# Attention and mixture of experts on one core: the attention loop re-ordered into two-step periods

## What is computed

```python
# q, k, v: (2, 8, 768, 64), proj: (64, 6)
q_bucket = sum(((q @ proj) > 0) * 2 ** arange(6));  k_bucket likewise
scores = q @ k.T / 8, set to -1e9 where q_bucket != k_bucket
attn = softmax(scores);  x = attn @ v            # 16 heads in all
x = moe(x, w_gate, w_noise, noise, w1, w2)       # 8 experts, the top 2 of each token
out = gelu_like(x @ w_in) @ w_out
```

## Time and profile before

| what | us |
|---|---|
| median of 3 executions (lowest, highest) | 1029.27 (1027.99, 1030.33) |
| profiled execution, its time / its span | 1037.7 / 1035.6 |
| TensorE matmul busy | 920.9 (89%) |
| VectorE / ScalarE / GpSimd busy | 428.7 / 348.8 / 416.7 |
| first transposes of step 0 / of step 12 / last normalise ends | 27.6 / 65.9 / about 304 |
| share of TensorE in the chain that ended last | 73% |

### The profile page before, as it was taken

How to read it: one execution, slowest core, us unless ns; L and a number is a source line. 1 busy time by engine, 2 the same in 40 slices (tenths; PEclk the granted TensorE clock), 3 DMA queues, 4 the chain that set the end, 5 groups by cost and what they waited for, 6 DMA issues and landing times.

```text
span 1035.6 us, 15081 instructions
## 1 busy us (share of the span) xinstructions
PE 920.9 (89%) x4789; PEld 746.9 (72%) x4790; DVE 428.7 (41%) x756; ACT 348.8 (34%) x616; POOL 416.7 (40%) x247
## 2 busy tenths in 40 slices
PE   3699999999975389969999999999389999999998
PEld 3566666666643368858888888888279999999996
DVE  4567776677535812212222222222354333333222
ACT  1576677666734011111111111111223232323222
POOL 1222110000028585799594857689695001000000
PEclk8899999999998589989999999999789999999999
DMA  7444653356014279744352525245432011000000
GB/s 161 114 123 110 159 137 85 94 138 168 1 76 162 81 254 343 242 151 155 112 165 94 162 81 172 89 154 162 134 130 82 21 51 38 33 0 0 31 1 31
DMA packets 73237, 116.45 MB, mean 112 GB/s; under 512 B 31920, under 2 KB 33968, under 8 KB 73200
## 3 DMA queue, kind: packets, MB, share of 16 engines
q1 hardware_dynamic: 60592, 86.61, 28.0%
q0 software_dynamic: 4400, 14.42, 4.8%
q10 hardware_dynamic: 8208, 14.95, 4.4%
HBM read 73.49 MB, written 23.59 MB: 94 GB/s over the span
## 4 chain that ended last, share of the span: by engine, by line
PE 73%; DVE 7%; POOL 7%; DMA 6%; SPq 2%; issue 2%; ACT 2%; POOLq 0%; ACTq 0%; DVEq 0%
PE psS L726 13%; PE psT L683 12%; PE psS L667 11%; PE psS L741 9%; PE psV L565 6%; PE psT L554 4%; PE psV L741 4%; PE psS L543 4%; POOL W L433 3%; POOL W L431 2%; DMA x_sb<-x_dram,gather_i 2%; DVE W L796 2%; PE psS L692 2%; PE psM L530 2%; DMA staged<-in_moe_w 2%
## 5 line engine op out<-in xcount | busy, mean ns | idle before, releaser
L431 POOL TENSOR_TENSOR W<-staged,ones_col 128x1024 fp32r<-128x1024 f32 x80 | 152.7, 1909 | 167.9 <-DMA staged<-in_moe_w 103.8
L433 POOL TENSOR_TENSOR W<-staged,W 128x1024 fp32r<-128x1024 f32 x80 | 192.8, 2410 | 6.3
L667 PE MATMUL psS<-W,xT_hi 128*128 x448 | 144.4, 403 | 2.0 <-DVE xT_lo L969 2.0
L726 PE MATMUL psS<-x2T_hi,W 128*128 (+1 forms) x512 | 134.0, 343 | 1.6 <-DVE x2T_lo L987 1.6
L683 PE MATMUL psT<-W,hT_hi 128*128 x448 | 124.5, 410 | 9.2 <-POOL W L433 9.2
L802 DVE TENSOR_REDUCE neg_max<-psS 128x1 f32<-128x768 f32 x96 | 91.6, 954 | 48.9 <-PE psS L543 48.0
L1038 ACT ACTIVATE prob<-psS,exp_arg 128x768 f32<-128x768 f32 x96 | 95.5, 994 | 32.8 <-DVE exp_arg L805 32.7
L543 PE MATMUL psS<-W 128*128 128x384 f32 x384 | 93.4, 366 | 10.7 <-DMA W<-k_hi 9.3
L726 PEld LDWEIGHTS psS<-x2T_hi,W 128*128 128x128 f32 x512 | 94.5, 191 | 6.8 <-issue 2.0
L683 PEld LDWEIGHTS psT<-W,hT_hi 128*128 128x128 f32 x448 | 81.2, 191 | 24.7 <-issue 9.4
L1047 ACT ACTIVATE probT<-psT 128x768 f32<-128x768 f32 x96 | 78.1, 813 | 61.0 <-PE psT L554 59.5
(11 more groups left out here) (170 smaller groups left out, 1295.2 us busy)
## 6 DMA issues: line engine op xcount, KB each, us to landing
staged<-in_moe_w SPq DMA_DIRECT2D x64, 512.0 KB, 3.5
xs_dram<-x_sb SPq DMA_DIRECT2D x31, 256.0 KB, 4.8
x_in<-xs_dram ACTq DMA_DIRECT2D x29, 256.0 KB, 2.7
ys_dram<-y_sb ACTq DMA_DIRECT2D x28, 256.0 KB, 2.4
W<-q_hi SPq DMA_DIRECT2D x32, 192.0 KB, 3.4
W<-k_hi SPq DMA_DIRECT2D x32, 192.0 KB, 3.7
staged<-in_moe_w_in SPq DMA_DIRECT2D x8, 512.0 KB, 3.6
staged<-in_moe_w_out SPq DMA_DIRECT2D x8, 512.0 KB, 3.4
```

The lines of the kernel that those rows point to most:

```text
L431: nc.gpsimd.tensor_tensor(W[:, at:at + CH], staged[:, n % 2], ones_col[:].to_broadcast([P, CH]), ALU.mult).then_inc(s_whi, 1)
L433: nc.gpsimd.tensor_tensor(W[:, at + BLOCK:at + BLOCK + CH], staged[:, n % 2], W[:, at:at + CH].bitcast(F32), ALU.subtract).then_inc(s_spli ...
L667: mm = nc.tensor.matmul(psS[:, 0, half], x[:, c * P:(c + 1) * P], W[:, bass.ds(slot + (w + c * F + half * 512), 512)], start=c == 0 and n ...
L726: mm = nc.tensor.matmul(psS[:, 0, f % 2, 0:GN], W[:, at:at + P], x[:, bass.ds(buf + c * GN, GN)], start=c == 0 and n == 0, stop=c == DC - ...
```

## The change

TensorE's and VectorE's orders are rewritten in periods of two steps, n even. On TensorE a period is: transposes of n, a unit, at a head's start `back`, `weighted`, transposes of n+1, scores of n+3, a unit, scores of n+4. On VectorE it is: statistics of n+2, `collect`, the unit of step n-1, `normalise`, the unit of step n, statistics of n+3. ScalarE keeps its order apart from where the units' copies fall. Units 0 to 3 of a pair move to the last four steps of the pair two before it, units 4 to 7 to steps 0, 2, 3 and 5 of the pair before it (the table `AHEAD`), and units 0 to 3 of pair 1 stand ahead of step 0's transposes. No instruction is added or removed, and the programs of SyncE and GpSimd are as before.

```diff
+        AHEAD = (-4, -3, -2, -1, 0, 2, 3, 5)
         def unit_at(n):
-            return n // PS + 1, n % PS
+            for pr in (n // PS + 1, n // PS + 2):
+                if pr < PAIRS and n - PS * (pr - 1) in AHEAD:
+                    return pr, AHEAD.index(n - PS * (pr - 1))
+            return None
...
         # tensor
             for n in range(2):
                 scores(n)
-            for n in range(STEPS):
+            for n in range(-4, 0):
+                unit(*unit_at(n))
+            transposes(0)
+            scores(2)
+            for n in range(0, STEPS, 2):
                 hd, t = divmod(n, NT)
-                if n + 2 < STEPS:
-                    scores(n + 2)
-                transposes(n)
-                pr, u = unit_at(n)
-                if pr < PAIRS and u < UNITS:
-                    unit(pr, u)
+                if n:
+                    transposes(n)
+                if unit_at(n):
+                    unit(*unit_at(n))
                 if t == 0 and hd >= 2:
                     back(hd - 2)
-                if t % 2 and hd:
+                if hd:
                     weighted(hd - 1, t // 2)
+                transposes(n + 1)
+                if n + 3 < STEPS:
+                    scores(n + 3)
+                if unit_at(n + 1):
+                    unit(*unit_at(n + 1))
+                if n + 4 < STEPS:
+                    scores(n + 4)
...
         # vector
-            for n in range(STEPS):
+            for n in range(-4, -1):
+                unit(*unit_at(n))
+            for n in range(0, STEPS, 2):
                 hd, t = divmod(n, NT)
+                if n + 2 < STEPS:
+                    statistics(n + 2)
                 if t == 0 and hd >= 2:
                     collect(hd - 2)
-                if t == 1 and hd >= 2:
+                if unit_at(n - 1):
+                    unit(*unit_at(n - 1))
+                if t == 0 and hd >= 2:
                     normalise(hd - 2)
-                if n:
-                    pr, u = unit_at(n - 1)
-                    if pr < PAIRS and u < UNITS:
-                        unit(pr, u)
-                if n + 2 < STEPS:
-                    statistics(n + 2)
+                if unit_at(n):
+                    unit(*unit_at(n))
                 if t == 2 and hd:
                     denominators(hd - 1)
+                if n + 3 < STEPS:
+                    statistics(n + 3)
```

More of the change, by code:

```diff
@@ L1056, in _ @@
                 evac(n)
-                pr, u = unit_at(n)
-                if pr < PAIRS and u < 4:
-                    unit(pr, u)
+                if unit_at(n) and unit_at(n)[1] < 4:
+                    unit(*unit_at(n))
             attention_over(act)
```

## The result

The changed kernel takes 1074.12 us (median of 4 executions, 1065.88 to 1078.97), the kernel before 1029.8 in the same comparison: a ratio of 1.042, 95% interval 1.034 to 1.049. The forecast was 1073 in 1060 to 1090. The total came out within 1.2 us, but not by the forecast's own sum: it left out a term of 13.9 us, and terms that it had too high made up for it. The four executions of the changed kernel lie 13 us apart, and those of before 6.

The account below looks back on a forecast made before the run. TensorE was taken to set the attention's pace, with new waits behind VectorE's strict order. Front 12.8, pairs 1 and 2 12.0, pairs 3 to 5 12.0, pair 6 2.0, pair 7 4.6: 43.4 on 1029.3 gives 1073, range 1060 to 1090.

Parts of the forecast that it names:

- Offset 0: Periods are named by their first step's offset in the pair; this one, the pair's start: 8.1 to 8.2 us, 5.42 before.
- offset 4: Period without a head's start or units 0 to 3: falls from 5.80 to 4.85 us, one lump fitting in its slack.
- The circle: At offset 4, scores, reduction, exponential, evacuation, transposes and next scores form a 4.83 us latency that takes back the 0.57 gain.
- +4.0: Added us per pair, 37.9 against 33.9, from the six periods' waits; counted for pairs 1 to 5.
- rival 2: TensorE's clock falls at 14 heads' starts, some 1.5 us each, +21 in all: 1094 us; chance 0.12.
- late q: Scaled q reaches unit 0, now four steps earlier, 2.7 us late; 2.0 counted in pairs 1 and 2, 2.5 at the front.
- Front: Four units ahead of step 0 put T(0) at 42.1 and step 12 at 78.7 against 65.9: +12.8 us.
- The end: Last pairs of the attention: pair 6, without units 0 to 3, +2.0 us; pair 7, with two heads' starts, +4.6.
- Faster: Rival 3: VectorE's statistics are over before T(n), so waits at offsets 0, 6 and 10 go: about 1025 us; chance 0.03.
- little change: Rival 4: half the heads' waits overlap the 4.83 latency, leaving part of the front's cost: 1029 to 1045 us; chance 0.05.
- q in time: The forecast's waits without lateness of the scaled q: 1066 us; chance 0.14.
- rival 1: The chunk lands sooner or GpSimd is ahead, so scaled q is not late: 1066 us; chance 0.14.

Follow-up runs that it names:

- the fillers: The changed kernel with useless transposes of the identity put on TensorE in the waits at each head's start: 1065.34 us, ratio 1.034 to the kernel before.
- Turning GpSimd's order: GpSimd scales the next pair's q ahead of splitting the weight chunk: 1064.84 us in the changed kernel, 1025.3 in the kernel before.
- the split of `weighted`: The kernel before with `weighted` cut into six pieces, one a step, and the last two units a step later: 1019.83 us, ratio 0.989.

## Why the prediction was right, and where not

- **Right, and shown: what sets the time.** The heads' starts. Undone alone they give back 32 us of the 44.5, their falls of the clock with them. VectorE kept its written order in the rows shown, so `collect` did wait behind the statistics.
- **Right in size: each period's waits**, where the clock held. Offset 0 8.2 forecast, 7.8 measured; 2: 5.43, 5.35; 4: 4.85, 4.83; 6: 7.7, 7.5; 8: 5.1, 5.04; 10: 6.65, 6.33. At offset 4 the number was right, and the reason was not: 4.83 is TensorE's own work with a lump in it, 90.27 to 95.10 in the timeline without a wait. The circle from scores over exponential and evacuation to transposes, forecast at 4.83, shows in the plain periods of pair 7, and is 4.70:

```profile
304.19 0.82 PE L559 MATMUL psT<-ident,prob 128*128 128x128 f32 x6
...
306.80 0.85 PE L559 MATMUL psT<-ident,prob 128*128 128x128 f32 x6 [0.34 <-ACT probT L1065]
...
308.89 0.82 PE L559 MATMUL psT<-ident,prob 128*128 128x128 f32 x6
```

  The second transposes wait 0.34 for the evacuation, the first no longer. A plain period is thus 0.15 shorter than before, not the same. Each of offsets 0, 6 and 10 was forecast 0.2 to 0.4 high: statistics hold VectorE for 1.07 (154.44 to 155.51) where 1.18 was counted, and a copy for 0.47 (to 155.98) where it was 0.56. So without falls a pair is +3.0 (7.8 + 5.35 + 4.83 + 7.5 + 5.03 + 6.33 = 36.8), not the **+4.0** of the sum.
- **Wrong: the clock, a term that the sum does not have.** It stood as rival 2, with 0.12 and 14 falls at 1.5. The profiled execution shows 9 falls of 1.3 to 1.7, 13.9 us, and the fillers take them away with the waits left in place. The row on which I had set it aside, 298 to 304 with 1.00, had 1.36 us idle in 6.0 in short pieces; the heads' starts idle for 2.3 in 7.8 (rival 2 had said 3 in 8.2).
- **Wrong: late q in pairs 1 and 2, 2.0 each.** Nothing in pair 1, 0.2 in pair 2. The chain took 10.8 us instead of 13.5, as the chunk landed sooner, and the slower head ahead of it left more time. The mechanism is real: it appears with 2.87 as soon as the heads' wait is gone, and with 10.8 and 13.0 us periods when the table stands alone. In pair 0 it was +1.95 (6.99 for 5.04), where I had 2.5.
- **Front +12.8: measured +11.2**, T(0) at 41.98 for 42.1. That start was right by luck: the first unit came at 35.0 where 36.1 was counted, and the units were 2.0 to 2.2 us apart where 1.85 was. And the four units ahead of T(0) are only half of the reason: without them step 12 is 4 us later still. What binds the front is the scaled q, twice: that of pair 1 at 35 us and that of pair 2 at offset 8. Turning GpSimd's order is worth 7.5.
- **The end: +2.0 and +4.6 forecast, +2.8 and +4.7 measured**, but with one fall of the clock in each, 1.7 and 1.4; the waits alone are +1.1 and +3.3.
- **The prediction's own figures.** The 4.28 us of TensorE's own work in a period of before should be 4.44 (see the split of `weighted`). In the changed order it is 4.36, the 4.70 of a plain period less its wait of 0.34. The bounds given for the single terms add up to 1060 to 1079, not to 1062 to 1084, and halfway to rival 2 is 1084, not 1090; the measured 1074 lies inside either way.
- **Rivals.** Faster, little change, and q in time are out as the whole story; rival 1's condition held for pairs 1 and 2.

The measured terms add up: 11.2 + 4.4 + 4.7 + 5.9 + 4.7 + 6.1 + 2.8 + 4.7 = 44.5. In the forecast the missing falls (-13.9) met too much late q (+4) and too long waits in pairs 1 to 5 (about +5), at the front (+1.6) and in pairs 6 and 7 (+2.2). That these nearly cancel, so that the total is 1 us off, is luck; what the forecast had earned is the place and the rough size of each wait.

What stays open: why the clock fell in 9 of the 14 heads' starts and not in the other 5, which have the same waits (with pair 1's units at their old places it fell in 6 of 14); and how often it fell in the other three executions, whose mean granted clock was 0.936 to 0.945 with spans of 1077.0 to 1063.9, the higher clock with the shorter span.

## What to carry to other kernels

Before moving a consumer next to its producer on one engine, walk the round trip through the other engines in their written order: what stands ahead of the answer there (here the statistics of a later step) is part of the wait. A single bank that is written, read, transposed back and written again should have other work between each pair of its users. When an order is tightened, look also at the queues that weren't touched: a step moved four places earlier inherits every load that was in time before.

## What the runs showed of the hardware that was not expected

Waits of 1.5 and 0.7 us in one period of 7.8 were enough, in three of six pairs, for TensorE's granted clock to fall from the 2.4 GHz to the 1.2 GHz level; at the odd heads' starts, with waits of 1.1 and 1.5, it fell in five of six pairs. Each time 1.3 to 1.7 us were lost in the work behind (`weighted` 2.83 us for 1.51, transposes 1.54 for 0.87). With 8 to 10 useless transposes of the identity (0.11 us each) in the same waits the granted clock was 1.00 in every period after step 12, and the attention ended 11.7 us earlier. In this kernel a wait on TensorE thus had two prices, its length and what comes behind it. The Trainium skill, TensorE: Matmul & The Clock Gate, "What's actually happening", says that the default is the throttled clock and that activity releases it; the fillers agree, 1.00 in every head's start instead of 0.80 to 0.82 in nine.
